# Leading halves of q and k by casting transfers from GpSimd's queue, and q's scale moved into the exponential, in an attention and two-expert-layer kernel

## The chip, the cores and the metric

The kernel runs on one core of one Trainium2 chip. The metric is the device time of one execution in microseconds. Before the change it is 911.62 us, the median of 3 runs (910.39 to 913.48). All arrays are float32 at the kernel's border.

## The reference

The input is attention with a decay per key, then two expert layers, each of which sends a token to one of eight experts. Only the attention is touched by the change:

```
q, k, v: (4, 8, 576, 64)    f: (4, 8, 576)
scores = (1 / sqrt(64)) * q @ k^T
cum    = cumsum(log(clip(f, 1e-4, 1)))
scores = scores + cum[query] - cum[key], and -1e9 where key > query
attn   = softmax(scores) over the keys
out    = attn @ v                    -> x: (2304, 512)
x      = experts(x); x = experts(x)  top 1 of 8, 512 -> 1024 -> 512
```

The term of the query's own cum is the same for all keys of a row and falls out of the softmax, so the kernel never adds it.

## The kernel before, in words

The 32 heads (4 batches of 8) are worked one after another, in a software pipeline written out by hand: while head h has its probabilities and its output computed, head h+1 has its scores computed by query to find each row's extreme value, and head h+2 has its operands prepared. Each engine has its own program with the same loop over h, and semaphores join them.

A product in float32r keeps fewer bits of each factor than float32, so q and k are each split in a leading part (hi, the value cast to float32r) and a rest (lo, the value less hi). The score is a sum of two matrix products: kB against qB (66 or 97 rows: hi of k against hi of q, and extra rows for the decay `cum` and for the row's extreme value), and kA against qA (128 rows: lo of k with hi of q stacked on hi of k with lo of q). There are three buffers each of qA, kA, qB, kB, used by h modulo 3, and two each of the raw loads.

Preparing head m = h+2 in iteration h, before the change:

- SyncE loads q and k twice each, once into the upper and once into the lower 64 partitions (`load_qk`, L271 to L275): four transfers of 144 KB.
- VectorE casts k into kA (`leading_k`, L779 to L784), 128 x 576. This is its first work of the iteration, before `routing_step` and `mins(n, 4)`.
- GpSimd copies the upper half of that into kB (`copy_k`, L1164 to L1167), ahead of `clear(h, 0)`.
- VectorE subtracts: k less its leading part into kA (`rest_k`, L793 to L797), between `mins(n, 3)` and `mins(n, 2)`.
- ScalarE multiplies q by the scale and casts (`leading_q`, L614 to L619), between `exps(h, 2)` and `exps(h, 3)`; GpSimd copies the upper half into qB (`copy_q`, L1159 to L1162), between `clear(h, 2)` and `clear(h, 3)`.
- VectorE subtracts for q (`rest_q`, L786 to L791), after `mins(n, 0)`.

The scale is negative (SCALE = -1/8), so the scores are held with their sign turned: `mins` (L817 to L825) adds the mask and takes a minimum of each row, five tiles a head, and `exps` (L621 to L626) applies the exponential with scale -1. The row of minima is transposed by TensorE (`minima_row`, L394 to L399) and written by ScalarE into a row of qB (`row_in`, L628 to L631), which releases `by_key(h+1, 0)`, the first matrix product of the next iteration. GpSimd zeroes the part above the diagonal of each block of probabilities (`clear`, L1169 to L1175); `weighted(h, t)` (L401 to L410) waits for that. `back` (L412 to L416) transposes the output of head h-1 and waits for all five `mins` of head h+1.

TensorE's order in an iteration is: by_key 0, by_key 1, by_query(n, 4), by_key 2, by_query(n, 3), weighted 0, by_key 3, by_query(n, 2), by_key 4, by_query(n, 1), by_query(n, 0), weighted 1, back, minima_row, weighted 2 to 4.

Other work shares the engines in some iterations. From h = 17 on, at the end of every odd iteration, ScalarE and VectorE split one eighth of the first expert's weights (`split_hi` L653, `split_lo` L990 with L993), and SyncE loads such an eighth (512 KB) in every even one from h = 16. `routing_step` (L1002) puts a few small operations of a finished batch on VectorE. GpSimd scatters table entries by an indirect transfer (`scatter`, L1210 to L1217, L1215) in iterations 17 to 21 and 25 to 29, after `clear(h, 4)`. At the start GpSimd builds constants, then the fixed rows of the buffers (`operand_rows`, L1177 to L1186); its semaphore s_pool counts these stages, and TensorE's 56 warm-up products wait for the first stage, SyncE's `load_c(1)`, tau and gate weights for the second.

Of the kernel before, what the change touches and what calls it, by code (L numbers as in the profile page):

```python
# [5 lines left out]
F32 = mybir.dt.float32  # L6
# [8 lines left out]
P = 128  # L15
# [5 lines left out]
def attention_moe_moe(nc, q_t, k_t, v_p, f, emb_t, tau, w1a, w2a, wg, w1b, w2b, out):  # L21
# [19 lines left out]
    SCALE = -float(D) ** -0.5  # L41
# [12 lines left out]
    with ExitStack() as ctx:  # L54
# [64 lines left out]
        q_raw = [asb(f"q_raw{a}", [2 * D, S]) for a in range(2)]  # L119
        k_raw = [asb(f"k_raw{a}", [2 * D, S]) for a in range(2)]  # L120
# [73 lines left out]
        q_in, k_in, c_in, v_in = sems("q_in", 2), sems("k_in", 2), sems("c_in", 3), sems("v_in", 3)  # L194
        q_hi, k_hi, q_cp, k_cp, q_lo, k_lo = (sem(n) for n in ("q_hi", "k_hi", "q_cp", "k_cp", "q_lo", "k_lo"))
# [72 lines left out]
        def _(sp):  # L268
            sp.dma_start(logf, f_h).then_inc(s_f, 16)

            def load_qk(h):  # L271
                a = h % 2
                for side in range(2):
                    sp.dma_start(q_raw[a][side * D:(side + 1) * D, :], q_h[h]).then_inc(q_in[a], 16)
                    sp.dma_start(k_raw[a][side * D:(side + 1) * D, :], k_h[h]).then_inc(k_in[a], 16)  # L275
# [42 lines left out]
            for h in range(HEADS):  # L318
                if h + 2 < HEADS:
                    sp.wait_ge(q_lo, h + 1)  # L320
                    sp.wait_ge(k_lo, h + 1)
                    sp.wait_ge(q_cp, h + 1)
                    sp.wait_ge(k_cp, h + 1)
# [286 lines left out]
        def _(act):  # L610
# [3 lines left out]
            def leading_q(h):  # L614

                act.wait_ge(q_in[h % 2], (h // 2 + 1) * 32)
                if h >= 3:
                    act.wait_ge(t_done[QT - 1], h - 2)
                act.mul(qA[h % 3][:], q_raw[h % 2][:], SCALE).then_inc(q_hi, 1)  # L619

            def exps(h, t):  # L621
# [4 lines left out]
                               scale=-1.0).then_inc(exps_done, 1)  # L626
# [31 lines left out]
            leading_q(0)  # L658
            act.wait_ge(s_ln, 2)
            act.activation(sq_j[0:HEADS, 0, 0:1], logf[:, 0:1], ACT.Exp)  # L660
            leading_q(1)
            row_in(0)

            for h in range(HEADS):
# [6 lines left out]
                if h + 2 < HEADS:  # L671
                    leading_q(h + 2)
# [30 lines left out]
            for m in range(2):  # L703

                if m == 0:
                    act.wait_ge(g_ent_out, 16 * GT)
# [48 lines left out]
        def _(dve):  # L755
# [13 lines left out]
            dve.memset(qB[0][CUM:CUM + 2, :].bitcast(F32), 1.0)  # L769
# [9 lines left out]
            def leading_k(h):  # L779

                dve.wait_ge(k_in[h % 2], (h // 2 + 1) * 32)
                if h >= 3:
                    dve.wait_ge(t_done[QT - 1], h - 2)
# [563 lines left out]
```

## Time and profile before

| what | before |
|---|---|
| median of the runs | 911.62 us |
| the profiled execution's own time | 915.94 us |
| its span, first to last instruction | 914.4 us |
| attention, all heads (to about) | 270 us |
| first expert layer begins at about | 300 us |
| TensorE busy in the span | 95% |
| VectorE, ScalarE, GpSimd busy | 61%, 44%, 32% |

The profiled execution is one run. What lies outside its span is 1.5 us. Matrix products are pipelined and their ends are modelled, so the share of TensorE is no proof that it never waits. A number in brackets behind an instruction in a timeline is the idle time of its engine before it, and behind the arrow stands what ended it.

### The profile page before, as it was taken

To read this page: it belongs to the slowest core of one execution; us is meant where nothing else is said; L and a number is where in the kernel's file an instruction comes from. 1 tells how busy PE (TensorE), PEld (TensorE's weight loads), DVE (VectorE), ACT (ScalarE), POOL (GpSimd) and SP (SyncE) were. 2 spreads that over 40 slices of the span, in tenths; PEclk is the share of its full clock that TensorE was granted. 3 is DMA by queue.
4 is the path that set the end of the run, shared out by engine and by line. 5 is a ranking of instruction groups with operands and counts; after the bars stand their busy time and mean duration, and the time that the engine had idled before them with its cause. 6 is when DMAs were issued, how large, how long until landed. Compare 5 with 4: busy or idle time off the path is not lost.

```text
span 914.4 us, 16446 instructions
## 1 busy us (share of the span) xinstructions
PE 868.5 (95%) x5092; PEld 716.0 (78%) x5093; DVE 560.6 (61%) x1661; ACT 404.5 (44%) x708; POOL 292.0 (32%) x459
## 2 busy tenths in 40 slices
PE   6999999999994899999999999969999999999996
PEld 5888787777774688888888888867888888888884
DVE  6677788888752377566577776636562263426643
ACT  2555555665650444435256435305552253324542
POOL 7444344544525322232332232222221221222220
PEclk7999999999997999999999999989999999999998
DMA  4334444555500746253445552405553162516100
GB/s 133 94 104 129 126 125 120 174 150 148 148 29 27 272 166 220 68 191 99 147 155 173 176 203 87 159 25 201 190 195 120 47 212 63 204 40 218 47 24 24
DMA packets 59244, 119.64 MB, mean 131 GB/s; under 512 B 11934, under 2 KB 20638, under 8 KB 59204
## 3 DMA queue, kind: packets, MB, share of 16 engines
q1 hardware_dynamic: 49476, 96.90, 33.1%
q0 software_dynamic: 9440, 22.18, 7.4%
q8 instruction: 20, 0.33, 0.2%
q14 instruction: 20, 0.16, 0.1%
q10 hardware_dynamic: 288, 0.07, 0.0%
HBM read 104.14 MB, written 17.99 MB: 134 GB/s over the span
## 4 chain that ended last, share of the span: by engine, by line
PE 84%; DVE 6%; DMA 3%; issue 3%; SPq 1%; POOL 1%; ACT 0%; POOLq 0%; DVEq 0%; ACTq 0%
PE ps L589 27%; PE ps L560 26%; PE ps L420 8%; PE ps L407 7%; PE ps L415 4%; PE ps L378 2%; PE ps L448 2%; PE ps L379 2%; PE ps L391 2%; PE ps L390 2%; PE ps L425 2%; DVE ps L824 1%; DMA k_raw<-in_k 1%; DMA xg<-x,ent_next 1%; DVE kA L796 1%
## 5 line engine op out<-in xcount | busy, mean ns | idle before, releaser
L993 DVE TENSOR_TENSOR wlo<-stage,whi 128x1024 fp32r<-128x1024 f32 x136 | 160.0, 1221 | 31.4 <-ACT whi L656 26.1
L656 ACT CAST whi<-stage 128x1024 fp32r<-128x1024 f32 x136 | 133.7, 1057 | 0.0
L724 ACT ACTIVATE h_s<-ps 128x512 f32<-128x512 f32 x44 | 26.3, 599 | 220.5 <-PE ps L560 213.2
L407 PE MATMUL ps<-probT,v_s 128*65 128x448 f32 (+4 forms) x384 | 103.2, 391 | 1.6 <-POOL probT L1174 1.3
L589 PE MATMUL ps<-whi,hT_hi 128*128 128x512 f32 x352 | 100.3, 407 | 0.0
L589 PE MATMUL ps<-whi,hT_lo 128*128 128x512 f32 x352 | 99.1, 403 | 0.0
L560 PE MATMUL ps<-whi,xT_hi 128*128 128x512 f32 x352 | 95.2, 392 | 3.0 <-DVE xT_lo L1071 3.0
L589 PE MATMUL ps<-wlo,hT_hi 128*128 128x512 f32 x352 | 95.6, 394 | 0.0
L560 PE MATMUL ps<-whi,xT_lo 128*128 128x512 f32 x352 | 95.1, 392 | 0.0
L560 PE MATMUL ps<-wlo,xT_hi 128*128 128x512 f32 x352 | 95.0, 392 | 0.0
L824 DVE CUSTOM_DVE_ANT_0 ps<-ps,maskf 128x576 f32<-128x576 f32 (+4 forms) x160 | 75.6, 510 | 24.6 <-PE ps L379 23.9
L625 ACT ACTIVATE probT<-ps 128x576 f32<-128x576 f32 (+4 forms) x160 | 66.4, 436 | 39.0 <-PE ps L391 35.1
L560 PEld LDWEIGHTS ps<-whi,xT_hi 128*128 128x128 f32 x352 | 65.7, 188 | 18.4 <-ACT xT_hi L715 3.5
L589 PEld LDWEIGHTS ps<-wlo,hT_hi 128*128 128x128 f32 x352 | 66.7, 189 | 14.7
L560 PEld LDWEIGHTS ps<-wlo,xT_hi 128*128 128x128 f32 x352 | 66.1, 188 | 14.5
L560 PEld LDWEIGHTS ps<-whi,xT_lo 128*128 128x128 f32 x352 | 66.1, 188 | 14.4
L1103 DVE TENSOR_TENSOR hT_lo<-ps,hT_hi 128x512 fp32r<-128x512 f32 x44 | 30.4, 691 | 73.1 <-ACT hT_hi L731 72.8
L589 PEld LDWEIGHTS ps<-whi,hT_hi 128*128 128x128 f32 x352 | 63.3, 190 | 11.4
L589 PEld LDWEIGHTS ps<-whi,hT_lo 128*128 128x128 f32 x352 | 63.0, 188 | 11.6
L390 PE MATMUL ps<-qB,kB 97*128 97x288 f32 (+2 forms) x192 | 70.0, 372 | 0.3 <-ACT probT L625 0.3
L1245 POOL COPY ent_next<-ent_tab 128x4 int32 (+1 forms) x46 | 8.6, 186 | 191.7 <-DVE ent_mid L1072 190.2
L1119 DVE COPY y_idx<-ent_cur 128x1 int32<-128x1 int32 x44 | 6.7, 153 | 93.3 <-PE ps L589 93.2
(191 smaller groups left out, 1618.3 us busy)
## 6 DMA issues: line engine op xcount, KB each, us to landing
stage<-in_moe_w SPq DMA_DIRECT2D x128, 512.0 KB, 3.7
q_raw<-in_q SPq DMA_DIRECT2D x64, 144.0 KB, 3.1
k_raw<-in_k SPq DMA_DIRECT2D x64, 144.0 KB
v_s<-in_v SPq DMA_DIRECT2D x32, 162.5 KB, 2.3
x<-o_rows SPq DMA_DIRECT2D x8, 512.0 KB
kB<-cum_hl SPq DMA_DIRECT2D x64, 2.2 KB
table<-entry POOLq DMA_INDIRECT x44, 2.1
table<-tinit SPq DMA_DIRECT2D x2, 288.0 KB
```

Of the source, the lines that this page charges most:

```text
L390: pe.matmul(o, kB[a][0:ROW + 1, k0:k0 + P], qB[a][0:ROW + 1, lo:hi], start=True, stop=False)
L407: mm = pe.matmul(ps[0:D + 1, OT_AT + lo:OT_AT + hi], v_s[h % 3][:, t, :], probT[:, col:col + hi - lo], start=(t == 0), stop=(t == QT - 1 o ...
L415: mm = pe.matmul(back_ps[:, t, :], o_t[:, t * P:(t + 1) * P], i_emb[:, h % H, :], start=True, stop=True)
L420: mm = pe.transpose(bank[:, c * P:(c + 1) * P], src[:, c * P:(c + 1) * P], ident[:])
L560: mm = pe.matmul(h_ps[hf], x[:, c * P:(c + 1) * P], w1_sl(w[b], c, hf * 512, 512), start=(wi == 0 and c == 0), stop=(wi == 2 and c == DC - 1))
L589: mm = pe.matmul(y_ps, h[:, kk * P:(kk + 1) * P], w2_sl(w[b], kk), start=(hf == 0 and wi == 0 and kk == 0), stop=(hf == 1 and wi == 2 and ...
L625: act.activation(probT[0:M, PT_AT[t]:PT_AT[t] + S - t * P], ps[0:M, T_AT[t]:T_AT[t] + S - t * P], ACT.Exp, scale=-1.0).then_inc(exps_done, 1)
L656: act.copy(whi[b][:, c, :], stage[:, c, :]).then_inc(w_hi[c], 1)
L724: act.activation(h_s[:, 0:512], h_ps[0], ACT.Relu).then_inc(h_relu[0], 1)
L824: dve.tensor_tensor_reduce(out=tile, in0=tile, in1=maskf[0:M, at:at + q1], scale=1.0, scalar=LARGE, op0=ALU.add, op1=ALU.min, accum_out=sm ...
L993: dve.tensor_tensor(wlo[b][:, c, :], stage[:, c, :], whi[b][:, c, :].bitcast(F32), ALU.subtract).then_inc(w_lo[c], 1)
L1103: dve.tensor_tensor(hT_lo[:, 0:512], hT_ps[0], hT_hi[:, 0:512].bitcast(F32), ALU.subtract).then_inc(h_lo[0], 1)
```

## The change

- q and k are loaded raw once each, into one buffer kq_raw (k in the upper 64 partitions, q in the lower), on SyncE.
- The leading parts are no longer computed by an engine. GpSimd issues five transfers a head that read float32 from HBM and write float32r (a cast in the transfer): q into both halves of qA, k into kB, q into qB, k into the lower half of kA (`load_hi`). They stand in GpSimd's queue ahead of `clear(h, 0)`, and wait until the buffer's last reader, by_key(h-1, 4), is done. `leading_q`, `leading_k`, `copy_q` and `copy_k` are gone.
- `rest_q` and `rest_k` wait for the raw loads and for all five casting transfers (80 counts of one semaphore).
- q stays unscaled. The scale, now +1/8, is applied inside the exponential; the rows for cum hold -8 in place of 1; the mask and the row reduction turn their signs (minimum to maximum).
- At the start, `load_hi(0)` is GpSimd's first work, `load_hi(1)` stands before `operand_rows(1)`, `load_hi(2)` after `operand_rows(2)`.
- Two waits for the attention's last stores are added before the first expert layer, on ScalarE and VectorE, since the memory map shifts.

```diff
-    SCALE = -float(D) ** -0.5
+    SCALE = float(D) ** -0.5
...
-        q_raw = [asb(f"q_raw{a}", [2 * D, S]) for a in range(2)]
-        k_raw = [asb(f"k_raw{a}", [2 * D, S]) for a in range(2)]
+        kq_raw = [asb(f"kq_raw{a}", [2 * D, S]) for a in range(2)]
...
-                for side in range(2):
-                    sp.dma_start(q_raw[a][side * D:(side + 1) * D, :], q_h[h]).then_inc(q_in[a], 16)
-                    sp.dma_start(k_raw[a][side * D:(side + 1) * D, :], k_h[h]).then_inc(k_in[a], 16)
+                sp.dma_start(kq_raw[a][0:D, :], k_h[h]).then_inc(kq_in[a], 16)
+                sp.dma_start(kq_raw[a][D:2 * D, :], q_h[h]).then_inc(kq_in[a], 16)
...
-                pe.wait_ge(q_cp, h + 1)
+                pe.wait_ge(hi_in[h % 3], (h // 3 + 1) * 80)
                 pe.wait_ge(q_lo, h + 1)
-                pe.wait_ge(k_cp, h + 1)
...
-                               scale=-1.0).then_inc(exps_done, 1)
+                               scale=SCALE).then_inc(exps_done, 1)
...
                 if m == 0:
+                    act.wait_ge(x1_stored, 64 * B)
                     act.wait_ge(g_ent_out, 16 * GT)
...
             def rest_q(h):
 
-                dve.wait_ge(q_hi, h + 1)
+                dve.wait_ge(kq_in[h % 2], (h // 2 + 1) * 32)
+                dve.wait_ge(hi_in[h % 3], (h // 3 + 1) * 80)
                 hi = qA[h % 3][D:2 * D, :]
-                dve.scalar_tensor_tensor(out=hi, in0=q_raw[h % 2][D:2 * D, :], scalar=SCALE, in1=hi.bitcast(F32),
-                                         op0=ALU.mult, op1=ALU.subtract).then_inc(q_lo, 1)
+                dve.tensor_tensor(hi, kq_raw[h % 2][D:2 * D, :], hi.bitcast(F32), ALU.subtract).then_inc(q_lo, 1)
...
-                if m < HEADS:
-                    leading_k(m)
...
+                if m == 0:
+                    dve.wait_ge(x1_stored, 64 * B)
...
+            def load_hi(h):
+
+                a = h % 3
+                if h >= 3:
+                    pool.wait_ge(t_done[QT - 1], h - 2)
+                for side in range(2):
+                    pool.dma_start(qA[a][side * D:(side + 1) * D, :], q_h[h]).then_inc(hi_in[a], 16)
+                pool.dma_start(kB[a][0:D, 0:S], k_h[h]).then_inc(hi_in[a], 16)
+                pool.dma_start(qB[a][0:D, :], q_h[h]).then_inc(hi_in[a], 16)
+                pool.dma_start(kA[a][D:2 * D, 0:S], k_h[h]).then_inc(hi_in[a], 16)
+
+            load_hi(0)
             pool.memset(ident[:], 0.0)
...
+            load_hi(1)
             operand_rows(1)
-            copy_q(0)
-            copy_k(0)
             operand_rows(2)
-            copy_q(1)
-            copy_k(1)
+            load_hi(2)
...
             for h in range(HEADS):
                 b, hh = h // H, h % H
-                if h + 2 < HEADS:
-                    copy_k(h + 2)
+                if 1 <= h < HEADS - 2:
+                    load_hi(h + 2)
                 clear(h, 0)
                 clear(h, 1)
                 clear(h, 2)
-                if h + 2 < HEADS:
-                    copy_q(h + 2)
                 clear(h, 3)
                 clear(h, 4)
```

## Rows read from the trace of the kernel before

**Rows 1.** The page's first part: busy time, share of the span and instructions of each engine.

```profile
PE 868.5 (95%) x5092; PEld 716.0 (78%) x5093; DVE 560.6 (61%) x1661; ACT 404.5 (44%) x708; POOL 292.0 (32%) x459
```

**Rows 2.** Timeline of ScalarE: when the row of minima of a head is written.

```profile
28.38 0.63 ACT L631 CAST qB<-ps 1x576 fp32r<-1x576 f32 x1 [1.28 <-PE ps L397]
...
158.04 0.63 ACT L631 CAST qB<-ps 1x576 fp32r<-1x576 f32 x1 [1.80 <-PE ps L397]
166.64 0.63 ACT L631 CAST qB<-ps 1x576 fp32r<-1x576 f32 x1 [2.83 <-PE ps L397]
...
254.33 0.63 ACT L631 CAST qB<-ps 1x576 fp32r<-1x576 f32 x1 [0.83 <-PE ps L397]
261.89 0.63 ACT L631 CAST qB<-ps 1x576 fp32r<-1x576 f32 x1 [2.38 <-PE ps L397]
```

**Rows 3.** Busy time by stretch, two iterations (12 and 18), with granted clock, DMA share, GB/s.

```profile
120.36:127.89 7.53, 7.53 (x54) 6.10 (x52) 6.23 (x23) 4.51 (x10) 3.14 (x7) 1.00 0.36 102
...
159.00:167.50 8.50, 8.06 (x52) 6.03 (x52) 7.62 (x23) 3.90 (x8) 4.05 (x8) 1.00 0.75 225
```

**Rows 4.** Timeline of iteration 12, which begins at 120.36 us and ends at 127.89.

```profile
121.93 0.73 POOL L1174 TENSOR_SCALAR_AFFINE_SELECT probT<-probT 128x128 f32<-128x128 f32 x2
...
122.73 1.13 PE L407 MATMUL ps<-probT,v_s 128*65 128x128 f32 x4
...
123.48 0.75 DVE L796 TENSOR_TENSOR kA<-k_raw,kB 64x576 fp32r<-64x576 f32 x1
...
124.71 0.48 POOL L1174 TENSOR_SCALAR_AFFINE_SELECT probT<-probT 128x128 f32<-128x128 f32 x2
...
125.53 1.19 PEld L415 LDWEIGHTS ps<-i_emb,o_t 65*128 65x128 f32 x10 [0.54 <-DVE smin L824]
```

**Rows 5.** Groups of instructions by line: the four that the change takes out.

```profile
L1162 POOL CAST qB<-qA 64x576 fp32r<-64x576 f32 x32 | 31.8, 994 | 7.5 <-ACT qA L619 6.9 <-POOL kB L1184 0.3
...
L1167 POOL CAST kB<-kA 64x576 fp32r<-64x576 f32 x32 | 22.1, 689 | 94.0 <-DVE kA L784 94.0
L619 ACT ACTIVATE qA<-q_raw 128x576 fp32r<-128x576 f32 x32 | 21.6, 676 | 1.2 <-DMA q_raw<-in_q 1.2
...
L784 DVE CAST kA<-k_raw 128x576 fp32r<-128x576 f32 x32 | 15.2, 474 | 4.1 <-DMA k_raw<-in_k 1.7 <-DVE lg_raw L875 1.7
```

**Rows 6.** The critical chain, part of iterations 17 and 18.

```profile
158.84 1.22 DVE wlo L993
160.05 0.38 DVE kA L784
160.43 0.06 issue
160.49 0.66 POOL kB L1167
```

**Rows 7.** GpSimd's transfers: plain load of a table (L263), then scatter (L1215), ns min/median/max.

```profile
L263 POOL DMA_DIRECT2D ent_tab<-table x16: 572/592/602, 294.7 to 858.5; - x16
...
DMA to landing us min/median/max: 1.7/2.3/5.5
...
L1215 POOL DMA_INDIRECT table<-entry x20: 969/1022/1547, 156.3 to 291.3; - x20
```

**Rows 8.** Timeline at 309 us, in the first expert layer.

```profile
309.01 2.36 DVE L993 TENSOR_TENSOR wlo<-stage,whi 128x1024 fp32r<-128x1024 f32 x2 [3.92 <-issue]
...
309.36 0.60 POOL L263 DMA_DIRECT2D ent_tab<-table  x1
```

**Rows 9.** The critical chain at 195 us: landing of a raw load behind a 512 KB load.

```profile
195.65 3.53 DMA k_raw<-in_k
```

**Rows 10.** Timeline of the start.

```profile
4.23 6.11 PE L448 MATMUL ps<-onesb,identb 128*128 128x128 bf16 x56 [4.23 <-DVE kB L772]
...
6.90 0.82 DVE L784 CAST kA<-k_raw 128x576 fp32r<-128x576 f32 x1 [1.73 <-DMA k_raw<-in_k]
...
13.13 0.37 PE L378 MATMUL ps<-kB,qB 66*128 66x288 f32 x1 [2.79 <-DMA kB<-cum_hl]
```

More of the change, by code:

```diff
@@ L192, in attention_moe_moe @@
         held = sem("held")
-        q_in, k_in, c_in, v_in = sems("q_in", 2), sems("k_in", 2), sems("c_in", 3), sems("v_in", 3)
-        q_hi, k_hi, q_cp, k_cp, q_lo, k_lo = (sem(n) for n in ("q_hi", "k_hi", "q_cp", "k_cp", "q_lo", "k_lo"))
+        kq_in, hi_in, c_in, v_in = sems("kq_in", 2), sems("hi_in", 3), sems("c_in", 3), sems("v_in", 3)
+        q_lo, k_lo = sem("q_lo"), sem("k_lo")
         s_done, t_done = sems("s_done", QT), sems("t_done", QT)
@@ L670, in _ @@
                 exps(h, 2)
-                if h + 2 < HEADS:
-                    leading_q(h + 2)
                 exps(h, 3)
@@ L768, in _ @@
             link(dve.memset(qB[0][D:P, :].bitcast(F32), 0.0), dve.memset(kB[0][D:P, :].bitcast(F32), 0.0))
-            dve.memset(qB[0][CUM:CUM + 2, :].bitcast(F32), 1.0)
+            dve.memset(qB[0][CUM:CUM + 2, :].bitcast(F32), -1.0 / SCALE)
             dve.memset(kB[0][ROW:ROW + 1, :].bitcast(F32), -1.0)
@@ L777, in _ @@
             dve.sem_inc(s_ln, 1)
[L779 to L783, printed above, removed]
-                dve.tensor_copy(kA[h % 3][:, 0:S], k_raw[h % 2][:]).then_inc(k_hi, 1)
             def rest_q(h):
-                dve.wait_ge(q_hi, h + 1)
+                dve.wait_ge(kq_in[h % 2], (h // 2 + 1) * 32)
+                dve.wait_ge(hi_in[h % 3], (h // 3 + 1) * 80)
                 hi = qA[h % 3][D:2 * D, :]
-                dve.scalar_tensor_tensor(out=hi, in0=q_raw[h % 2][D:2 * D, :], scalar=SCALE, in1=hi.bitcast(F32),
-                                         op0=ALU.mult, op1=ALU.subtract).then_inc(q_lo, 1)
+                dve.tensor_tensor(hi, kq_raw[h % 2][D:2 * D, :], hi.bitcast(F32), ALU.subtract).then_inc(q_lo, 1)
             def rest_k(h):
-                dve.wait_ge(k_cp, h + 1)
-                dve.tensor_tensor(kA[h % 3][0:D, 0:S], k_raw[h % 2][0:D, :], kB[h % 3][0:D, 0:S].bitcast(F32),
+                dve.wait_ge(kq_in[h % 2], (h // 2 + 1) * 32)
+                dve.wait_ge(hi_in[h % 3], (h // 3 + 1) * 80)
+                dve.tensor_tensor(kA[h % 3][0:D, 0:S], kq_raw[h % 2][0:D, :], kB[h % 3][0:D, 0:S].bitcast(F32),
                                   ALU.subtract).then_inc(k_lo, 1)
-            leading_k(0)
             dve.wait_ge(s_ln, 2)
@@ L805, in _ @@
             rest_k(0)
-            leading_k(1)
             dve.wait_ge(s_pool, 1)
@@ L823, in mins @@
                 at = S - P + M - q1
-                dve.tensor_tensor_reduce(out=tile, in0=tile, in1=maskf[0:M, at:at + q1], scale=1.0, scalar=LARGE, op0=ALU.add,
-                                         op1=ALU.min, accum_out=smin[0:M, j:j + 1]).then_inc(mins_done, 1)
+                dve.tensor_tensor_reduce(out=tile, in0=tile, in1=maskf[0:M, at:at + q1], scale=1.0, scalar=-LARGE, op0=ALU.add,
+                                         op1=ALU.max, accum_out=smin[0:M, j:j + 1]).then_inc(mins_done, 1)
             def embeddings():
@@ L1079, in _ @@
             for m in range(2):
-                if m == 1:
+                if m == 0:
+                    dve.wait_ge(x1_stored, 64 * B)
+                else:
                     dve.wait_ge(y_out, tile.get(16, 16))
@@ L1150, in _ @@
             plink(pool.memset(onesb[:], 1.0))
-            pool.affine_select(out=maskf[:, S - P:S], in_=maskf[:, S - P:S], compare_op=ALU.is_ge, fill=MASKED, base=0,
+            pool.affine_select(out=maskf[:, S - P:S], in_=maskf[:, S - P:S], compare_op=ALU.is_ge, fill=-MASKED, base=0,
                                pattern=[[-1, P]], channel_multiplier=1)
```

18 lines of the change are left out of this document (1 added, 17 removed).

## The prediction

> **What bounds the kernel now.** I read first the page's busy shares [rows 1]: TensorE 95%, VectorE 61%, ScalarE 44%, GpSimd 32%. That says that taking work off the last three is worth nothing by itself; it pays only where TensorE waits for them. The change touches the attention alone, some 270 of the 914.4 us. So the next view is the timeline of the one instruction that ends each head's preparation, the row of minima on ScalarE [rows 2]: its distances are the periods of the heads. The last is 261.89 - 254.33 = 7.56 us, and most others are the same, so this is the period at which TensorE alone sets the pace: the windows of iteration 12 [rows 3] show it busy for 7.53 of 7.53 us at granted clock 1.00. From 28.38 to 261.89 there are 30 periods in 233.51 us; 30 x 7.54 would be 226.2. The excess is 7.3 us. Three of the periods hold the products of the ranks (about 0.34 us each, TensorE's own work), so **6.2 us is all that waiting costs in the steady part**, and it lies in some ten iterations from 16 on. The worst is 166.64 - 158.04 = 8.60 us, an excess of 1.06. The windows of that iteration [rows 3] show VectorE busy 7.62 of 8.50 us, and the chain [rows 6] goes: the weights' split (1.22 us), VectorE's cast of k, GpSimd's copy of k, and behind it the first clear, for which TensorE waits.
>
> **What goes.** Per head: VectorE 0.474, ScalarE 0.676, GpSimd 0.689 + 0.994 us [rows 5]. In the 20 undisturbed iterations none of it is on the path: TensorE has no gap, so I cost their removal there at nothing; what covers it is TensorE's own 7.53 us. The one idle spell there, 0.54 us of the weight loader before `back` [rows 4], lies under the products of `weighted` 1 that still run. In the disturbed even iterations (18, 20, 22, 24, 26, 28; excess 1.06, 0.32, 0.74, 0.92, 1.05, 0.32, together 4.4) the chain of [rows 6] loses its second and fourth piece: clears no longer depend on VectorE, and `mins` move 0.47 us forward (more where small operations of the routing sat blocked beside GpSimd's copy). I leave about 0.3 us in each of the six, 1.8 in all. The other 1.8 us (iterations 9, 15, 17, 23 and 25, 0.35 to 0.37 each) is either the same 0.47 us or a raw load that landed late because SyncE issued four; it issues two now, and they are needed three microseconds later in the iteration. Removed: 6.2 - 1.8 = 4.4, less a bit for what I can't see: **-4.2 us**. Evidence that the removal is enough: the iteration that ends at 261.89 has the split too, but no operands left to prepare, and it takes 7.56.
>
> The change of signs and scale costs nothing: an exponential with scale 1/8 and a maximum have the form of what they replace, and the subtraction for q loses a multiplication in an instruction as long as the one for k, 0.75 us [rows 4]. The two waits for stores before the expert layer cost nothing: the stores are issued long before the last of the 20 table scatters (its start is 291.3 in [rows 7]), for which ScalarE waits anyway. SyncE loses 64 of 128 issues.
>
> **What comes: five transfers a head on GpSimd.** This is what decides. The price of one on GpSimd is not in the trace; the nearest rows [rows 7] are a plain load of 128 rows, 0.59 us in all 16 cases, and an indirect scatter, 1.02 (to 1.55). The new transfers are plain in form and have 64 rows, so I take 0.6 and keep 1.02 as the other end; below 0.59 only a little, since that row hardly varies. Beside a VectorE subtraction of two SBUF inputs the plain load still took 0.60 [rows 8], so I add nothing for that. The Trainium skill ("DMA: Bandwidth & Descriptors", at-a-glance table) puts the first byte of a GpSimd transfer at about 1 us for the emission; with that as the price of each issue the sum would be the second rival's, near 935 us. The rows for the form at hand say 0.59, and the sum goes by them.
>
> Where they lie, counted from the start of an iteration (120.36 in [rows 4]): the last clear ends at 125.19, which is 2.7 us before the next iteration's start. `load_hi` runs from there: 5 x 0.6 = 3.0, to +0.3. The first clear begins at +1.57 (121.93), so nothing is late for it. Landing: 2.3 us from issue (1.7 to 5.5) [rows 7] for 36 KB; for 144 KB I take 2.6. The last transfer is issued at -0.3 and lands at **+2.3**. `rest_k` starts at +3.12 (123.48) and has some 0.3 us of slack before `back` and the row of maxima go late (0.54 us of loader idle, less TensorE's own remainder). So in plain iterations there is about 1.1 us to spare: no cost, and no gain.
>
> In iterations 18 to 22 and 26 to 29 a scatter of the previous iteration comes first: 0.4 us of gap and 1.0 to 1.55 of issue. `load_hi` then begins at -1.2, its last issue is at +1.2, the landing at **+3.8**, and later where the 512 KB load of even iterations is under way (a raw load behind one took 3.53 us [rows 9], so about +0.9). VectorE waits in order in front of `rest_k`, with three `mins`, `rest_q` and the norm queued behind it, and TensorE waits for these in `back`. Against a limit of +3.4 that is 0.4 us late in the four odd ones and 1.3 in the five even ones, where I have left 0.3 already: 4 x 0.4 + 5 x 1.0 = 6.6 at these values, 0 with the shortest landing (1.7). Half the landings seen are below 2.3, and VectorE is itself behind after a split, so I take **+3.5 us**.
>
> **The start.** GpSimd issues `load_hi(0)` first: 3.0 us later for all its stages. TensorE's warm-up (6.1 us for 56 products) began at 4.23 [rows 10] and would begin at about 6.5 and end at 12.5. The first scores began at 13.13, when the rows of cum had landed; VectorE's scan waited for the cast of k (6.90 to 7.72) before it, and without the cast cum lands near 11.4. So warm-up is the later, 12.5: **-0.6 us**. GpSimd's second stage (constants 2.3 us, `load_hi(1)` 3.0, fixed rows about 3.5 more) ends at 12.8; what hangs on it (load of the gate weights, needed by the embeddings at about 17.5) still comes in time, so it costs nothing. With 1.02 in place of 0.6 these stages are 2.1 and 4.2 us later.
>
> Traffic: seven transfers of 144 KB a head in place of four, 0.43 MB more per 7.54 us, 57 GB/s on top of 102 to 225 [rows 3]. It fits if a cast packet costs what a plain one does.
>
> **Sum.** -4.2 + 3.5 - 0.6 = -1.3 us. Made against the profiled execution (915.94, span 914.4), it gives 914.6; that run lies 4.3 above the median, and I carry the difference to the median: **910.3 us**. A measurement here tells about 0.3%, 2.7 us, from no change.
>
> **The rivals.**
> 1. *The landings come in time everywhere*, and TensorE, no longer idle between warm-up and first scores, isn't slowed there. Then the 3.5 goes and up to 1.5 more is saved: 905 to 908. For it: landings of 1.7 us, VectorE's own lateness. Against: 15 transfers' worth of room is gone after each scatter. Chance 0.22.
> 2. *Slower: GpSimd becomes the pace.* The place is GpSimd's queue between `clear(h-1, 4)` and `clear(h, 0)`. The point from which it decides is 0.85 us per issue: then the last landing is at -2.7 + 3.4 + 2.6 = +3.3, the limit, in every iteration. At 1.02: issues end at +2.4, 0.5 past the limit of the first clear; the last lands at +4.0, 0.6 late, x 21 = 12; after a scatter 2.1 x 9 = 19; less 4 and plus 3 at the start: 30 over the rest, about 940; at 0.9 about 922. For it: every other GpSimd transfer in the trace costs about 1 us, and a cast has to be set up. Against: the plain form's 0.59. Chance 0.25.
> 3. *A casting packet takes the DMA engines twice as long.* Five then take 3.7 us of transfer behind each other and land at +2.9 in plain iterations, +4.7 after a scatter: 3 to 10 us slower, 914 to 920. Nothing in the trace shows a casting packet. Chance 0.10.
> 4. *The change doesn't do what it says*: casting transfers that share a semaphore run one behind another, five landings of 2.3 us, 11.5 a head, +120 us. Against: the scatters share one too and follow each other faster than they land. Chance 0.03.
>
> **Numbers.** The forecast has 0.40, its own range 907.5 to 913. Over 0.3% faster than 911.62 is below 908.9: 0.12 of the forecast and rival 1, 0.34. Slower, above 914.4: 0.03 of the forecast and rivals 2, 3, 4, 0.41. Within: 0.25. The range leaves a tenth out on each side: 906 to 932.
>
> **What would show it.** In the changed kernel's profile: GpSimd's transfers at 0.6 us each (rival 2: 0.85 and more); VectorE idle before L796's successor, released by a transfer, only in iterations 18 to 22 and 26 to 29 (rivals 2 and 3: everywhere); period 7.54 in the early heads; the iteration of 8.60 us down to about 7.9; first scores at 12.5. I am wrong if the early heads' period moves off 7.54 in any direction: up is rival 2 or 3, down would mean that TensorE was not the pace there.

## The result, and the profile after

The changed kernel takes **955.38 us** (median of four runs, 952.16 to 961.05), against 911.96 for the kernel before: a ratio of 1.0466 (95% interval 1.0442 to 1.049), 43 us slower. The forecast was 910.3 and its range ended at 932. The profiled execution of the changed kernel took 961.05 us (span 959.4), 45.1 us more than the one before (915.94).

The page of the changed kernel, first its busy time by engine as in [rows 1], then its DMA queues (packets, MB, share of the 16 engines' span; q1 is SyncE's, q0 GpSimd's):

```profile
PE 884.7 (92%) x5092; PEld 731.4 (76%) x5093; DVE 540.0 (56%) x1629; ACT 386.3 (40%) x676; POOL 318.7 (33%) x555
...
q1 hardware_dynamic: 44356, 87.46, 28.4%
q0 software_dynamic: 22240, 45.78, 18.3%
```

VectorE lost 20.6 us of work and ScalarE 18.2 (the groups taken from them in [rows 5] are 15.2 and 21.6); GpSimd gained 26.7, since its issues count. TensorE executes the same 5092 products and is busy 16.2 us longer: the same work at a lower clock.

The timeline of ScalarE, the row of maxima of each head, which answers to [rows 2] (start, duration; in brackets the idle time before it and what ended it):

```profile
156.74 0.63 ACT L619 CAST qB<-ps 1x576 fp32r<-1x576 f32 x1 [2.38 <-PE ps L392]
164.27 0.63 ACT L619 CAST qB<-ps 1x576 fp32r<-1x576 f32 x1 [1.45 <-PE ps L392]
178.32 0.63 ACT L619 CAST qB<-ps 1x576 fp32r<-1x576 f32 x1 [8.81 <-PE ps L392]
187.37 0.63 ACT L619 CAST qB<-ps 1x576 fp32r<-1x576 f32 x1 [0.23 <-PE ps L392]
...
306.91 0.63 ACT L619 CAST qB<-ps 1x576 fp32r<-1x576 f32 x1 [2.38 <-PE ps L392]
```

The row that was at 261.89 is now at 306.91: 45.0 us later, so the whole loss of 45.1 lies in the attention. Most periods are 7.54 still (164.27 - 156.74 = 7.53), but iteration 18 takes 178.32 - 164.27 = 14.05 us and iteration 19 takes 9.05. The 30 periods that end at 306.91 have an excess over 30 x 7.54 of 51.8 us, where [rows 2] had 7.3. Ten of them, 18 to 23 and 26 to 29, take 119.8 us in place of 75.4: 44.4 of the 51.8.

The waits of the changed kernel from 20 to 310 us (total, times, longest):

```profile
PEld ps L410 <- DVE smin L801: 47.7, 30, 6.6
DVE kA L775 <- DMA kA<-in_k: 33.0, 9, 6.2
PE ps L410 <- DVE smin L801: 29.3, 8, 5.9
```

L775 is `rest_k`, the subtraction that makes the trailing part of k (L796 before). VectorE waits nine times, 33.0 us in all, for the last of the five casting transfers, and TensorE then waits in `back` for the minima (now maxima, L801) that are queued behind it. The timeline of iteration 18, GpSimd, SyncE's queue and VectorE:

```profile
162.87 1.46 POOL L1192 DMA_INDIRECT table<-entry  x1 [0.69 <-issue]
164.31 1.14 POOL L1130 DMA_DIRECT2D qA<-in_q  x2
165.24 0.33 SPq L281 DMA_DIRECT2D v_s<-in_v  x1
...
165.62 0.43 SPq L291 DMA_DIRECT2D stage<-in_moe_w  x1
...
166.09 0.43 SPq L299 DMA_DIRECT2D x<-o_rows  x1
166.38 0.61 POOL L1133 DMA_DIRECT2D kA<-in_k  x1
...
166.89 1.05 POOL L1153 TENSOR_SCALAR_AFFINE_SELECT probT<-probT 128x128 f32<-128x128 f32 x3
167.19 1.07 SPq L272 DMA_DIRECT2D kq_raw<-in_k  x1
...
173.63 0.75 DVE L775 TENSOR_TENSOR kA<-kq_raw,kB 64x576 fp32r<-64x576 f32 x1 [5.21 <-DMA kA<-in_k]
```

The clears begin at 166.89, and in [rows 4] the first clear begins 1.57 us after the iteration does; so the iteration begins near 165.3, and the last transfer is issued at +1.1. The prediction had +1.2. But it lands at 173.5 (the chain of waits of the changed kernel):

```profile
166.38 7.16 DMA kA<-in_k
...
175.40 2.41 PE ps L410 x10
```

That is **7.2 us from issue to landing, where the prediction took 2.6** (3.5 behind a 512 KB load). Busy time by stretch of the same iteration, as in [rows 3] (length, then TensorE, its loader, VectorE, ScalarE, GpSimd; granted clock, DMA share, GB/s):

```profile
166.00:168.00 2.00, 2.00 (x13) 1.50 (x12) 1.90 (x8) 1.36 (x3) 1.83 (x5) 1.00 1.01 235
168.00:170.00 2.00, 2.00 (x14) 1.47 (x12) 0.42 (x2) 0.55 (x2) 0.52 (x2) 1.00 0.91 263
170.00:172.00 2.00, 0.49 (x2) 0.00 (x0) 0.00 (x0) 0.00 (x0) 1.61 (x3) 1.00 1.08 329
172.00:174.00 2.00, 0.00 (x0) 0.00 (x0) 0.37 (x1) 0.00 (x0) 2.00 (x5) 1.00 1.19 363
174.00:176.00 2.00, 0.60 (x3) 0.60 (x4) 1.97 (x8) 0.00 (x0) 0.05 (x1) 0.66 1.45 253
176.00:178.00 2.00, 2.00 (x14) 2.00 (x14) 0.28 (x2) 0.00 (x0) 0.00 (x0) 0.50 0.33 60
178.00:180.00 2.00, 2.00 (x10) 1.22 (x7) 1.00 (x5) 0.63 (x1) 0.00 (x0) 0.50 0.00 0
180.00:182.00 2.00, 2.00 (x11) 1.94 (x11) 0.00 (x0) 1.32 (x3) 0.00 (x0) 0.63 0.34 88
```

Two things are to be seen. The DMA share (the packets' times added up, as a share of the 16 engines; it can pass 1, and it is no rate, since 1.08 goes with 329 GB/s in one window and 1.01 with 235 in another) is 0.91 to 1.45 from 166 to 176. The 0.75 of [rows 3] is a mean over iteration 18. In the kernel before, single windows of that iteration were as full, but with nothing in GpSimd's queue that VectorE waited for:

```profile
163.00:165.00 2.00, 1.78 (x11) 1.01 (x11) 1.97 (x10) 0.49 (x2) 1.29 (x3) 1.00 1.04 338
```

And after TensorE has stood from about 170.5 to 175.4, its granted clock is 0.50 (1.2 of 2.4 GHz), until about 181.5; the stall is paid a second time in the products that follow.

Which queue the engines served is in the DMA view of the changed kernel. First from 61 to 64 us, where the five transfers of a plain iteration (one without a scatter ahead of them) run all but alone (total of the 3 us), then from 168 to 172 (total of the 4 us):

```profile
q0 software_dynamic: 370, 0.70, 111.8%
...
q1 hardware_dynamic: 486, 0.87, 70.3%
q0 software_dynamic: 171, 0.32, 29.2%
```

Alone, GpSimd's queue moves 0.70 / 3 = 0.23 MB per us, and the five transfers (0.74 MB) are through in about 3.2 us. Beside SyncE's queue it gets 0.32 / 4 = 0.08, a third of that. That the company of SyncE's transfers makes the landing late is tested below (loads_after_hi, weights_early), and the section on the prediction comes back to it. Over the whole kernel the last transfer's issue and landing read (count, issue in ns as minimum/median/maximum; then the landing in us):

```profile
L1133 POOL DMA_DIRECT2D kA<-in_k x32: 529/554/607, 3.8 to 284.6; - x32
...
DMA to landing us min/median/max: 3.0/3.7/8.3
```

The start, to set beside [rows 10]:

```profile
6.71 5.23 PE L443 MATMUL ps<-onesb,identb 128*128 128x128 bf16 x56 [6.71 <-POOLq L1146]
...
9.17 5.05 SPq L277 DMA_DIRECT2D kB<-cum_hl  x4
...
13.62 0.37 PE L373 MATMUL ps<-kB,qB 66*128 66x288 f32 x1 [1.67 <-DMA kB<-cum_hl]
```

### The profile page after: what moved, and what is told of

Same layout as the page of the kernel before. It is cut to its first block, busy times and chain, and to the rows that moved or that the text cites. A ratio compares the mean times of both kernels' runs of the same rounds, so it can differ in the third digit from the quotient of the medians.

```text
span 959.4 us, 16404 instructions
## 1 busy us (share of the span) xinstructions
PE 884.7 (92%) x5092; PEld 731.4 (76%) x5093; DVE 540.0 (56%) x1629; ACT 386.3 (40%) x676; POOL 318.7 (33%) x555
## 4 chain that ended last, share of the span: by engine, by line
PE 81%; DMA 8%; POOL 4%; DVE 3%; issue 2%; ACT 1%; POOLq 0%; DVEq 0%; SPq 0%; ACTq 0%
PE ps L584 26%; PE ps L555 25%; PE ps L415 7%; PE ps L402 7%; DMA kA<-in_k 5%; PE ps L410 4%; PE ps L385 2%; PE ps L386 2%; PE ps L373 2%; PE ps L443 2%; PE ps L374 2%; PE ps L420 2%; POOL table L1192 1%; POOL qA L1130 1%; PE ps L392 1%
## 5 line engine op out<-in xcount | busy, mean ns | idle before, releaser
L402 PE MATMUL ps<-probT,v_s 128*65 128x448 f32 (+4 forms) x384 | 109.5, 411 | 1.1 <-POOL probT L1153 1.1
L801 DVE CUSTOM_DVE_ANT_0 ps<-ps,maskf 128x576 f32<-128x576 f32 (+4 forms) x160 | 75.2, 511 | 53.5 <-PE ps L374 51.7
L1153 POOL TENSOR_SCALAR_AFFINE_SELECT probT<-probT 128x128 f32<-128x128 f32 (+1 forms) x160 | 45.0, 284 | 144.8 <-ACT probT L613 139.4
L410 PEld LDWEIGHTS ps<-i_emb,o_t 65*128 65x128 f32 x320 | 43.3, 213 | 49.7 <-DVE smin L801 47.7
L410 PE MATMUL ps<-i_emb,o_t 65*128 65x73 f32 x320 | 46.6, 299 | 30.8 <-DVE smin L801 29.3
L385 PE MATMUL ps<-qB,kB 97*128 97x288 f32 (+2 forms) x192 | 73.6, 389 | 0.3 <-ACT probT L613 0.3
L584 PEld LDWEIGHTS ps<-whi,hT_lo 128*128 128x128 f32 x352 | 63.0, 189 | 11.5
```

The source lines that it names most:

```text
L385: pe.matmul(o, kB[a][0:ROW + 1, k0:k0 + P], qB[a][0:ROW + 1, lo:hi], start=True, stop=False)
L402: mm = pe.matmul(ps[0:D + 1, OT_AT + lo:OT_AT + hi], v_s[h % 3][:, t, :], probT[:, col:col + hi - lo], start=(t == 0), stop=(t == QT - 1 o ...
L410: mm = pe.matmul(back_ps[:, t, :], o_t[:, t * P:(t + 1) * P], i_emb[:, h % H, :], start=True, stop=True)
L584: mm = pe.matmul(y_ps, h[:, kk * P:(kk + 1) * P], w2_sl(w[b], kk), start=(hf == 0 and wi == 0 and kk == 0), stop=(hf == 1 and wi == 2 and ...
L801: dve.tensor_tensor_reduce(out=tile, in0=tile, in1=maskf[0:M, at:at + q1], scale=1.0, scalar=-LARGE, op0=ALU.add, op1=ALU.max, accum_out=s ...
L1153: pool.affine_select(out=block, in_=block, compare_op=ALU.is_ge, fill=0.0, base=0, pattern=[[1, M]], channel_multiplier=-1).then_inc(clear ...
```

## The experiments

**Two theories.** A: the five transfers land too late for `rest_k`, where VectorE waits in order; whatever gives the landing more lead, or moves the waiting instruction back, gives the time back. B: the added work itself costs the time (GpSimd's issues, 14 MB more traffic, the other arithmetic), wherever it lies; then more lead changes little.

### four_buffers: one head more of lead

```diff
-        qA = [asb(f"qA{a}", [2 * D, S], F32R) for a in range(3)]
+        qA = [asb(f"qA{a}", [2 * D, S], F32R) for a in range(4)]
...
-                    pool.wait_ge(t_done[QT - 1], h - 2)
+                    pool.wait_ge(t_done[QT - 1], h - 3)
...
-                if 1 <= h < HEADS - 2:
-                    load_hi(h + 2)
+                if 1 <= h < HEADS - 3:
+                    load_hi(h + 3)
```

(kA, qB, kB and their semaphores likewise; the fourth buffer's fixed rows are filled by GpSimd in iteration 1, and the embeddings' norms move into iteration 0.)

> The changed kernel with four buffers of qA, kA, qB, kB in place of three, and the five casting transfers of head h+3 issued in iteration h, one head earlier than its subtractions need them. Bytes, issues and order of the engines' work stay. Theory A (the transfers are issued too close to their use: the fifth lands 7.2 to 8.3 us after issue in iterations 18, 20, 22, 26 and 28, and needs to be there about 4 us after it): all waits of the k subtraction for a transfer vanish (33 us in the changed kernel), TensorE's clock doesn't fall in the loop, and the time is 905 to 913. Rival B (the DMA engines can't carry seven transfers a head beside weights and stores, whatever the lead): the waits move or stay, 935 to 955. Two us may be lost once at the start for the fixed rows of the fourth buffer.

Measured: 917.36 us (median of ten, one of which took 2521.86 us for no cause that the record shows, and is not in the ratio) against 915.68 beside it, ratio 1.0021 (0.9999 to 1.0043). That is above the 905 to 913 expected of theory A and far below the 935 of its rival. In the waits of this kernel `rest_k` never waits for a casting transfer, and only twice for a raw load:

```profile
DVE kA L777 <- DMA kq_raw<-in_q: 2.9, 2, 2.2
```

The same 32 x 5 casting transfers, the same bytes and the same arithmetic, and of the loss of 4.7% there is 0.2% left. A holds, and B falls as the main cause. The periods of iterations 0 to 3 are 9.23, 8.55, 9.60 and 9.07 us here, 36.5 us together where the kernel before takes 32.7, so about 4 us are lost at the start, where the fourth buffer is filled; 2 were expected.

### signs_only: the arithmetic alone

The kernel before, with the sign and the scale changed and maximum for minimum (in the subtraction for q, the fixed rows and the mask too), and nothing else:

```diff
-    SCALE = -float(D) ** -0.5
+    SCALE = float(D) ** -0.5
...
-                act.mul(qA[h % 3][:], q_raw[h % 2][:], SCALE).then_inc(q_hi, 1)
+                act.mul(qA[h % 3][:], q_raw[h % 2][:], 1.0).then_inc(q_hi, 1)
...
-                               scale=-1.0).then_inc(exps_done, 1)
+                               scale=SCALE).then_inc(exps_done, 1)
...
-                                         op1=ALU.min, accum_out=smin[0:M, j:j + 1]).then_inc(mins_done, 1)
+                                         op1=ALU.max, accum_out=smin[0:M, j:j + 1]).then_inc(mins_done, 1)
```

> The kernel before with the change of sign and scale alone: q unscaled, the exponential with scale 1/8, mask and row reduction turned to maximum, -8 in the rows for cum; loads, casts and copies as before. All theories: no change, ratio to before 0.997 to 1.003; if it were slower, part of the 43 us would be the arithmetic's.

Measured: 912.42 us against 913.81, ratio 0.9978 (0.9959 to 0.9997). It costs nothing.

### scatter_in_middle: the scatter no longer ahead of the five

In the changed kernel, the scatter of the routing table stood behind `clear(h, 4)`, directly ahead of the next `load_hi`; here `clear(h, 3)`, `clear(h, 4)` and the norms go behind it.

```diff
                 clear(h, 2)
+                if b > 1 and 1 <= hh <= QT:
+                    if b == 2:
+                        pool.wait_ge(s_init, 64)
+                    scatter(b - 2, range(hh - 1, hh))
                 clear(h, 3)
                 clear(h, 4)
                 if b > 0 and hh == 6:
                     norms(b - 1)
-                if b > 1 and 1 <= hh <= QT:
-                    if b == 2:
-                        pool.wait_ge(s_init, 64)
-                    scatter(b - 2, range(hh - 1, hh))
```

> The changed kernel, but the table scatter of iterations 17 to 21 and 25 to 29 stands between the third and fourth clear in place of behind the fifth, so that it doesn't delay the next casting transfers. Theory A: all five are issued before SyncE's 512 KB load starts, as in iteration 24, which has the load, no scatter before it and no wait; the five waits of 5 to 6 us vanish, time 912 to 922. Rival B (the engines are overloaded in every even iteration): waits of several us stay, above 935. The fourth clear may come 1 us late, up to 5 us in all.

Measured, one execution: 930.34 us, between theory A's 912 to 922 and the rival's 935. `rest_k` waits (the waits of this kernel)

```profile
DVE kA L775 <- DMA kA<-in_k: 12.4, 7, 4.8
```

12.4 us in place of 33.0, and 20.6 us less of waiting made the profiled execution 30.7 us shorter. Of the five long waits, which were all to vanish, one stayed, 4.8 us in iteration 22 (the one with a weight load and the stores), those of 18 and 20 shrank to 1.35 and 0.76, and those of 26 and 28 went; iteration 15 waits 1.94 us as before the edit (1.96), where no scatter but the norms stand ahead of the five.

### rest_k_last: the waiting instruction behind the maxima

```diff
-                if m < HEADS:
-                    rest_k(m)
...
+                    rest_k(m)
```

(`rest_k(h + 2)` moves behind the last of the iteration's `mins`, so that nothing TensorE needs in this iteration stands behind it.)

> The changed kernel, but the subtraction for k stands behind the last of the five maxima in place of behind the second. Theory A (VectorE waits in order, with three maxima behind it that TensorE needs in the same iteration): a landing that is late by up to 2 us costs nothing any more, the waits of iterations 1, 5, 13 and 15 have no effect; those of 5 to 6 us shrink to 2 to 4, since the operands are needed at the next iteration's first us. Time 925 to 940. Rival (the lateness itself, not what stands behind it, is the price): 950 to 956.

Measured, one execution: 924.90 us, just below the range expected (925 to 940), and in the waits of this kernel

```profile
DVE kA L775 <- DMA kA<-in_k: 16.6, 6, 3.9
```

Six waits, the longest 3.9 us: after some scatters the landing is late even against this later limit. Iteration 15, which waits 1.96 us in the changed kernel, takes 7.56 us here: a landing late by that much costs nothing once nothing stands behind the wait.

### loads_after_hi: SyncE's big transfers behind the five

SyncE waits for the five landings of the head before it issues the weight load and the stores of attention rows.

```diff
+                if 0 < h < HEADS - 2:
+                    sp.wait_ge(hi_in[(h + 2) % 3], ((h + 2) // 3 + 1) * 80)
```

> The changed kernel, but SyncE waits for the casting transfers of head h+2 before it issues the 512 KB weight load and the stores of iteration h. Theory A with its cause in the shared DMA engines (SyncE's load and stores run beside the last casting transfers and share the engines packet by packet): the wait of the k subtraction falls from 5.2 to 6.2 us to about 1 in the five iterations after a scatter, time 915 to 925. Rival C (GpSimd issues them too late, and the landing would be as late with empty engines): waits of 5 us stay, 950 to 956.

Measured, one execution: 935.74 us, where 915 to 925 was expected if the big transfers were the cause and 950 to 956 if not. The waits of VectorE and then of SyncE's queue:

```profile
DVE kA L777 <- DMA kA<-in_k: 19.1, 15, 3.1
...
SPq L272 <- DMA kA<-in_k: 56.8, 18, 5.6
```

The longest wait is halved (3.1 in place of 6.2), which says that the big transfers were part of each landing. But there are now 15 waits, and SyncE's own queue stood for 56.8 us at the raw load of k. The gain was partly given back through a new wait, so this run bounds the share of the big transfers only from one side.

### weights_early: the weight loads elsewhere

The eight early weight loads of 512 KB, of even iterations from 16 on, go to iterations 2 to 9.

```diff
-                if h >= HEADS - 2 * H and (h - HEADS) % 2 == 0:
-                    c = (h - (HEADS - 2 * H)) // 2
+                if 2 <= h < 2 + CH:
+                    c = h - 2
```

> The changed kernel with the eight 512 KB weight loads issued in iterations 2 to 9 in place of every even one from 16. The scatter stays where it is, and so do the stores of 576 KB (iterations 18, 22, 26). Theory A (only scatter and a big SyncE transfer together make the fifth landing 7 to 8 us late): the waits of iterations 20 and 28 vanish (6.1 and 5.5 us), those of 18, 22 and 26 shrink to 1 to 3 with the store alone, and iterations 2 to 9, which have no scatter before them, show no new wait over 1 us, as iteration 24 does; time 925 to 935. Rival (the scatter's own delay is enough): waits of 5 us stay in all five, 950 to 956.

Measured, one execution: 944.05 us, and 24.0 us of waits in ten. The expectation missed: 925 to 935 us was foreseen, with no stall in iterations 20 and 28 and 1 to 3 us in 18, 22 and 26, which wait 3.96, 4.17 and 4.24. The waits of 20 and 28 fell from 6.10 to 3.47 us and from 5.53 to 3.42. Iteration 20 in the timeline of this kernel, and its stretches:

```profile
185.34 0.60 POOL L1133 DMA_DIRECT2D kA<-in_k  x1
...
191.11 0.75 DVE L775 TENSOR_TENSOR kA<-kq_raw,kB 64x576 fp32r<-64x576 f32 x1 [3.47 <-DMA kA<-in_k]
```

```profile
186.00:188.00 2.00, 2.00 (x13) 1.49 (x12) 1.46 (x4) 0.75 (x2) 0.84 (x3) 1.00 1.24 278
188.00:190.00 2.00, 1.78 (x11) 1.00 (x10) 0.00 (x0) 1.75 (x6) 0.84 (x3) 1.00 1.01 177
```

With no weight load in the way the landing still takes 191.11 - 185.34 = 5.8 us, beside v and two raw loads (0.46 MB). So the scatter's delay together with SyncE's ordinary transfers makes about 3.5 us of lateness, and the 512 KB load adds 2.6 at iteration 20 and 2.1 at 28.

### three_tuned and four_tuned: the repair

`three_tuned` has both edits, rest_k_last and scatter_in_middle, and the changed kernel's three buffers. `four_tuned` has four buffers as well, whose fixed rows SyncE copies from the third.

> The changed kernel with its three buffers, with the k subtraction after the five maxima and the scatter between the third and fourth clear. Each alone left 5 to 6 late heads at other places. Theory A (each covers what the other doesn't: the scatter no longer delays the issue, and 2 us of lateness no longer cost): ratio to before 0.997 to 1.005. Rival (iteration 22, with load, stores and late landing, stays): up to 1.010.

> Four buffers and casting transfers one head earlier, as in four_buffers; the fourth buffer's fixed rows are copied by four transfers of SyncE from the third in place of GpSimd's fills; the k subtraction stands after the five maxima; the scatter stands between the third and fourth clear. Theory A: start level with the kernel before within 1 us, the loop at 7.54 a head but for some 2 us, so 4 to 5 us less than before: ratio 0.994 to 0.998. Rival B (the extra traffic still slows single iterations): ratio 1.000 to 1.005.

Measured: `three_tuned` 910.10 us, ratio 0.9958 (0.9936 to 0.998) against 913.81 beside it; `four_tuned` **908.53 us, ratio 0.9921 (0.9899 to 0.9943)**. Both beat the kernel before, and both by a little more than expected (0.997 to 1.005 and 0.994 to 0.998). In `three_tuned` `rest_k` waits

```profile
DVE kA L775 <- DMA kA<-in_k: 2.5, 2, 2.2
```

2.5 us in all, where each edit alone left 12.4 and 16.6. The stretch from first to last row of maxima is 237.6 us here (clock 0.99, DMA share 0.79), where the kernel before needs 243.6 and the changed one 288.2:

```profile
18.75:256.36 237.61, 237.00 (x1614) 192.06 (x1615) 171.94 (x593) 117.87 (x256) 135.71 (x321) 0.99 0.79 190
```

Around the start of iteration 18 of `three_tuned` GpSimd's queue is nearly done before SyncE's starts (25 of its packets begin after 159 us, beside SyncE's); the DMA view from 156 to 159 us:

```profile
q0 software_dynamic: 375, 0.71, 114.7%
q1 hardware_dynamic: 1, 0.00, 0.3%
```

### before_rest_last: is it the order alone?

The kernel before, with `rest_k` moved behind the minima.

> The kernel before with its k subtraction moved after the five minima, nothing else. It asks whether the gain of the tuned variants is the transfers' or the order's. If the order's: up to 3 us less than before, ratio 0.996 to 0.999. If the late iterations before are bound by the cast and copy ahead of the first clear, as the chain said: ratio 0.999 to 1.001.

Measured: 913.02 us, ratio 0.9985 (0.9965 to 1.0004). `rest_k`'s place alone gives nothing that can be measured (the interval takes in most of both ranges expected); the even iterations from 18 on still take 8.14 to 8.20 us. Its rows of minima go from 18.24 to 260.16, 241.9 us; `three_tuned` is 4.3 us below that, which must come from the work that the change removes, or from the scatter's new place, which was not tried in the kernel before. Of the 4.3, 1.0 lies in iteration 0 (9.17 us against 10.15), ahead of the steady part.

### extra_plain and extra_cast: the price of five more transfers

The kernel before, with five transfers of 144 KB a head more on GpSimd, behind `clear(h, 4)`, into buffers that nobody reads. In `extra_plain` they are plain, in `extra_cast` the buffers are float32r, so that the transfers cast.

```diff
+        dummy = [asb(f"dummy{a}", [2 * D, S], F32) for a in range(3)]
...
+                    for i, src in enumerate((q_h, q_h, k_h, q_h, k_h)):
+                        lo = (i % 2) * D
+                        pool.dma_start(dummy[i // 2][lo:lo + D, :], src[h + 3]).then_inc(x_in, 16)
```

> The kernel before, with five more transfers a head on GpSimd after the last clear, from the same places of q and k and of the same size as the change's, float32 into spare float32 buffers that nobody reads: GpSimd's issue and the traffic of the change without its deadline. Theory A2 (what costs is that VectorE waits for the landing, not the issue or the bytes): 912 to 920, with GpSimd's first clear late only after a scatter; engine time per MB on GpSimd's queue near the 3.1 us that SyncE's queue has before. Rival B (bytes): over 925.

> As extra_plain, but the spare buffers are float32r, so that the five transfers cast. If a cast costs the DMA engines what a plain copy does: same landings and the same time as extra_plain within 0.3%. If it costs half as much again, as 4.6 against 3.1 us of engine time per MB in the changed kernel suggests: the fifth landing is 0.5 to 1.5 us later than with plain ones, the share of the engines higher at the same bytes; the time may still be the same, since nobody waits.

Not shown in the edit: GpSimd waits for the five landings of the head before ahead of each next five (1.3 us in all in `extra_plain`, 0.4 in `extra_cast`), and the two waits for the attention's last stores are added as in the change. With the condition on h the five are issued for 29 heads, 145 transfers.

Measured: `extra_plain` 921.69 us, ratio 1.0105 (1.0088 to 1.0122); `extra_cast` 924.63 us, ratio 1.0136 (1.0119 to 1.0153). The first is a little above the 912 to 920 expected, and below the 925 of the rival. Issues and queue of the plain one, then of the casting one (two views of each, the line's issues and the page's third part):

```profile
L1240 POOL DMA_DIRECT2D dummy<-in_k x58: 516/526/711, 27.9 to 251.4; - x58
...
q0 software_dynamic: 16400, 43.57, 15.8%
```

```profile
L1240 POOL DMA_DIRECT2D dummy<-in_k x58: 517/543/567, 28.5 to 251.3; - x58
...
q0 software_dynamic: 21040, 43.57, 17.4%
```

A casting transfer is issued as fast as a plain one (0.54 and 0.53 us). It costs the engines some 20% more time: over the 21.4 MB added, 17.4% of 921.8 us less the 7.4% of 914.4 that q0 had before is 92.7 us of all engines, 4.3 us per MB; for the plain ones 77.1 us, 3.6 per MB. The two differ in more than the cast: from the packets of q0 (9440 before) a plain transfer has 48 and a casting one 80, and the trace has the casting ones' data in packets of 2304 bytes, one row, and the plain ones' in packets of 4608. So it isn't shown how much of the 20% is the cast's and how much the smaller packets'. Here nobody waits for the transfers, and they cost 9 and 12 us on top of all the work of the kernel before. The early iterations keep their 7.54 us; the loop is 5 us longer, in iterations from 16 on. The profiled executions are 1.7 and 7.4 us above that of the kernel before, and what lies outside the loop was not followed up.

## Why the prediction was wrong

**The step that failed** is the landing after a scatter: "the landing at +3.8, and later where the 512 KB load of even iterations is under way (a raw load behind one took 3.53 us [rows 9], so about +0.9)". The place, the instruction and the issue times were right: the last issue came at +1.1 in iteration 18, foreseen at +1.2, and the long waits are all in the five even iterations that the prediction lists. The landing was 7.2 us behind it, not 2.6 or 3.5, so `rest_k` waited 5.2 us, where I had 1.3 of lateness. I took the landing from the median of transfers of 36 KB, plus one row of a raw load behind a 512 KB load [rows 9]. That treats the engines as free, and a big transfer as a fixed delay. The slowest of those 36 KB landings, the 5.5 us in [rows 7], spoke against it: it is that of the issue in [rows 8], beside a 512 KB weight load (the DMA view of the kernel before, 309 to 311 us):

```profile
ent_tab<-table POOLq DMA_DIRECT2D x1, 36.0 KB, 5.5
```

In plain iterations too 2.6 was short, since the quickest of the 32 landings took 3.0 us and the median is 3.7; in iteration 5, whose five had the engines all but alone, the last landed 4.6 us after its issue, and the 1.1 us to spare was gone (a wait of 0.54).

The traffic was weighed only as a mean ("it fits"): over the early loop it does (DMA share 0.45 before, 0.72 after, from 60 to 140 us), but in the 9 us that begin at 164.3 the five transfers (0.74 MB) share the engines with v (0.17), a weight load (0.52), the stores (0.59) and two raw loads (0.29). That is 2.3 MB, and at the 235 to 363 GB/s of the windows it takes 6 to 10 us. One row already in hand spoke of it: DMA share 0.75 at 225 GB/s in iteration 18 [rows 3]. I read it as room for 57 GB/s. By windows of 2 us it is 0.93 and 1.04 from 161 to 165: engines that SyncE's queue keeps busy just when the five are due.

What made it worse is the order. Without a scatter GpSimd's queue runs ahead of SyncE's: alone for 3 us. One scatter (1.46 us here, with a gap of 0.7 ahead of it) puts the five at the same time as v, weights and stores, and the packets of both queues then pass in turn: 171 packets of GpSimd's against 486 of SyncE's from 168 to 172 us, and 36 against 66 from 191 to 192. GpSimd's rate falls to a third. The Trainium skill ("DMA: Bandwidth & Descriptors", section "Queues, rings and completion order") says that each DMA engine goes round the queues that have work and takes a whole packet, of several descriptors, from one before it switches. The trace agrees in kind: both queues move at once, and GpSimd's moves less than alone. It doesn't show the turns: SyncE's queue has 2.8 and 1.8 packets to one of GpSimd's in the two windows above, and the trace's packets, of one row of 2304 bytes for the five, need not be the page's. That rule asks for the bytes in flight to be added up, where I added a delay.

Bytes are not the whole of it. In iteration 20 there are no stores, and the landing still took 8.3 us:

```profile
190.00:192.00 2.00, 2.00 (x13) 1.50 (x12) 1.46 (x4) 0.81 (x2) 0.88 (x3) 1.00 1.06 280
...
194.00:196.00 2.00, 0.00 (x0) 0.00 (x0) 0.00 (x0) 0.08 (x1) 2.00 (x4) 1.00 0.81 147
```

The engines are at 0.81 while they move 147 GB/s. Why a busy engine moves less in that window stays open.

**The second failed term** is the price of a late microsecond. The prediction charged 1 us of lateness as 1 us. Measured, the five long waits are 28.7 us and the ten periods that hold them and follow them are 44.4 us over, 3.1 us more for each stall. The granted clock of 0.50 behind it accounts for that: in iteration 18 it stands from 175.4 to about 181.5, and 6.1 us at half speed is some 3 us lost (an estimate). The same in the repair: 20.6 us less of waiting was worth 30.7. Short waits are dear as well: those of 1.56 and 1.96 us in iterations 1 and 15 put the two periods from there on 2.90 and 3.35 us over, with a granted clock of 0.53 from 38 to 40 us and 0.50 from 148 to 150, while 0.54 us in iteration 5 cost 0.49.

**What was overlooked**: not only scatters stand ahead of `load_hi`. In iteration 14 the norms do (1.20 us on GpSimd at 136.19), the first of the five is issued at 137.35, and iteration 15 waits 1.96 us. Waits of 1.56, 0.54 and 0.24 us are in iterations 1, 5 and 13; why the landing was late there was not traced.

**What else came out otherwise.** The four odd iterations (19, 21, 27, 29) were to be 0.4 late each; none waits. The stall ahead of each lets GpSimd run on: the next five are issued by 174 us, while TensorE still stands, and `rest_k` of iteration 19 begins at 183.78. The first scores came at 13.62, half a microsecond later than in [rows 10] and not 0.6 earlier: the warm-up began at 6.71 and ended at 11.9, earlier than foreseen, but the rows of cum landed at about 13.6, later than the 11.4 I worked out.

**What was right.** The issue takes 0.53 to 0.57 us (0.6 taken), so rival 2, GpSimd as the pace (0.25), is out: the early periods stayed at 7.54. Rival 3, the casting packet twice as long (0.10), is out as put: 20% more engine time per MB. Rival 4 (0.03) is out: five landings one behind another would take 11.5 us, and the last of the five lands 3.7 us (median) behind its own issue. Rival 1 (0.22), landings in time everywhere, is the opposite of what came. Signs and scale cost nothing. The part removed is worth about what I said, and shows only where nothing waits: the loop of `three_tuned` is 6.0 us shorter than that of the kernel before. Of that, 0.9 is in iteration 0, so 5.1 in the 30 periods for which the -4.2 was reckoned, and before_rest_last has 1.7 of those by the order of `rest_k` alone. The iteration of 8.60 us (18) takes 156.51 to 164.05 there, 7.54 (7.9 was foreseen). So the removal is worth 3.3 to 5.1 us, as far as single profiled executions tell it, and part of that may be the scatter's new place: the -4.2 fits, but is not shown by itself. The +3.5 beside it should have been 45.0 + 4.2, about +49.

Of what was to show it, "VectorE idle only in 18 to 22 and 26 to 29" is true of the long waits and, of those iterations, of the even ones alone. The range ended too near, because the forecast and every rival were priced with landings on engines that have little else to do.

## What to carry to other kernels

Before moving loads to another queue, add up per iteration what all queues have in flight in the few microseconds in which the load must land, and divide by what the engines move when full; a mean share of DMA says nothing of that. An instruction that waits for a load should stand behind everything on its engine that the critical engine needs, and nothing of variable length should stand ahead of the load on its queue; both together turned a loss of 4.7% into a gain of 0.4%, and a fourth buffer made it 0.8%. Price a stall of TensorE above its length: here 3 us came on top of each wait of 5 to 6, and 1.3 to 1.4 on top of waits of 1.6 to 2.0.

## What the runs showed of the hardware

- A transfer of 64 rows x 2304 bytes on GpSimd's queue is issued in 0.53 us plain and 0.54 us casting; the casting one costs more at the engines, 4.3 against 3.6 us of all sixteen per MB, and moves in packets of 2304 bytes where the plain one's have 4608.
- GpSimd's queue moved 0.23 MB per us alone and 0.08 beside SyncE's queue with its weight load, stores and raw loads; the landing of the last of five went from 3.0 to 8.3 us.
- After TensorE had stood for about 5 us its granted clock was 0.50 in the windows that followed, and the next iteration took 9.05 us in place of 7.54. After a wait of 1.96 us it was 0.50 too (148 to 150 us), and the next iteration took 8.94.
